# Attention in a fused attention, dense and routed expert kernel: 64-row half turns, 64-row blocks of q and k, and a new order of steps

## The reference

```python
# attention: q, k, v of shape (4, 8, 576, 64)
scores = scale * np.matmul(q, k.transpose(0, 1, 3, 2))
mask = pos[:, None] // 64 >= pos[None, :] // 64        # block causal, block 64
scores = np.where(mask, scores, -1e9)
attn = np.exp(scores - scores.max(-1, keepdims=True))
attn = attn / (attn.sum(-1, keepdims=True) + 1e-09)
x = np.matmul(attn, v)                                 # then laid out as 2304 rows of 512
# dense layer: w_in 512 x 2048, w_out 2048 x 512
h = x @ w_in
x = np.where(h > 0, h, np.exp(np.minimum(h, 0)) - 1) @ w_out
# routed layer: rows with x @ w_skip > 0 go through one of 8 experts (512 x 1024 x 512), picked by argmax
out = x; out[r] += gate[r] * (np.maximum(x[r] @ w1[e], 0) @ w2[e])
```

## Time and profile before

| | |
|---|---|
| median of 3 runs | 821.57 us (820.05 to 821.72) |
| the profiled execution | 823.07 us |
| its span, first to last instruction | 821.0 us |
| TensorE busy | 796.7 us (97%), weight loads 661.8 us (81%) |
| DVE, ACT, POOL busy | 527.3 (64%), 341.0 (42%), 244.3 us (30%) |
| mean granted clock of TensorE | 0.992 of full speed |
| attention, about | the first 200 us of the span |

### The profile page before, as it was taken

One profiled execution on the slowest core, in us unless ns is written; L12 is line 12 of the kernel. 1 busy time (PEld: TensorE's weight loads), 2 busy tenths in 40 slices (PEclk: granted clock), 3 DMA queues, 4 the chain that ended last, 5 costly groups with the idle time before them and its releaser, 6 DMA issues.

```text
span 821.0 us, 14719 instructions
## 1 busy us (share of the span) xinstructions
PE 796.7 (97%) x4610; PEld 661.8 (81%) x4611; DVE 527.3 (64%) x1291; ACT 341.0 (42%) x830; POOL 244.3 (30%) x240
## 2 busy tenths in 40 slices
PE   6999999999999999999999999999997999999995
PEld 4777777778989988988888898889875777888884
DVE  3777777775333687588488578635656799367342
ACT  4666666654342222222322322233443676256141
POOL 3666676674560121021021012100112323213111
PEclk9999999999999999999999999999997999999999
DMA  8355565645332210200200010140342699164000
GB/s 156 108 148 145 155 157 158 179 128 170 104 105 97 87 53 28 87 21 11 77 20 20 28 51 26 52 154 26 126 140 67 216 343 345 74 225 148 20 27 8
DMA packets 102912, 88.09 MB, mean 107 GB/s; under 512 B 66676, under 2 KB 78340, under 8 KB 102736
## 3 DMA queue, kind: packets, MB, share of 16 engines
q1 hardware_dynamic: 97408, 81.89, 32.6%
q0 software_dynamic: 3056, 5.00, 1.9%
q10 hardware_dynamic: 2400, 0.59, 0.4%
HBM read 72.26 MB, written 18.34 MB: 110 GB/s over the span
## 4 chain that ended last, share of the span: by engine, by line
PE 77%; SPq 10%; issue 4%; DMA 3%; DVE 3%; ACT 1%; DVEq 1%; ACTq 0%; POOL 0%; POOLq 0%
PE h_ps L1707 12%; PE out_ps L1707 11%; PE h_ps L1708 11%; PE h_ps L1709 11%; PE out_ps L1709 11%; PE out_ps L1708 11%; SPq L229 4%; SPq L231 3%; DMA recip_rows<-r_rows 2%; PE o_ps L670 2%; PE t_ps L620 2%; SPq L268 2%; SPq L265 2%; PE out_ps L1843 1%; PE s_ps L612 1%
## 5 line engine op out<-in xcount | busy, mean ns | idle before, releaser
L1534 ACT ACTIVATE ex<-h_ps 128x384 f32<-128x384 f32 x96 | 47.2, 491 | 271.8 <-PE h_ps L1709 271.8
L1707 PE MATMUL h_ps<-xt_hi,wi_hi 128*128 128x384 f32 x384 | 131.7, 343 | 0.0
L1708 PE MATMUL h_ps<-xt_lo,wi_hi 128*128 128x384 f32 x384 | 129.8, 338 | 0.0
L1709 PE MATMUL h_ps<-xt_hi,wi_lo 128*128 128x384 f32 x384 | 129.7, 338 | 0.0
L1373 DVE TENSOR_SCALAR ex<-ex 128x384 f32<-128x384 f32 x96 | 36.1, 376 | 140.1 <-ACT ex L1534 139.0
L1707 PE MATMUL out_ps<-wo_hi,gt 128*128 128x512 f32 x288 | 114.5, 398 | 0.0
L1709 PE MATMUL out_ps<-wo_hi,gt 128*128 128x512 f32 x288 | 113.9, 396 | 0.0
L1708 PE MATMUL out_ps<-wo_lo,gt 128*128 128x512 f32 x288 | 113.3, 393 | 0.0
L520 ACT ACTIVATE prob<-s_ps,negmax 128x128 f32<-128x128 f32 (+2 forms) x144 | 77.8, 548 | 61.8 <-DVE negmax L389 56.3
L1255 DVE CUSTOM_DVE_ANT_0 x2t<-x,w_raw 128x512 bf16<-128x512 f32 x108 | 82.7, 806 | 0.4
L1151 POOL TENSOR_TENSOR xt_lo<-x_raw,xt_hi 128x384 fp32r<-128x384 f32 x20 | 28.4, 1418 | 157.2 <-ACT xt_hi L1549 157.1
(11 more groups left out here) (180 smaller groups left out, 1616.3 us busy)
## 6 DMA issues: line engine op xcount, KB each, us to landing
w_raw<-in_moe_w_dram SPq DMA_DIRECT2D x56, 512.0 KB, 5.2
attn_t<-attn_sb SPq DMA_DIRECT2D x16, 288.0 KB, 2.2
x_raw<-attn_t SPq DMA_DIRECT2D x24, 192.0 KB, 2.4
out_dram<-x SPq DMA_DIRECT2D x18, 256.0 KB, 2.2
x_rows<-x SPq DMA_DIRECT2D x18, 256.0 KB, 2.5
raw_qk<-in_q_dram SPq DMA_DIRECT2D x32, 128.0 KB, 2.5
v<-in_v_dram SPq DMA_DIRECT2D x32, 128.0 KB, 2.7
wi_raw<-in_moe_w_in_dram SPq DMA_DIRECT2D x16, 256.0 KB, 2.8
```

The lines of the kernel that those rows point to most:

```text
L1534: act.activation(ex[:, f % 2], h_ps[:, f % 2, 0:NB], ACT.Exp).then_inc(ex_done, 1)
L1707: pe.matmul(dst, stat[0], mov[0], start=start, stop=False, skip_group_check=True)
L1708: pe.matmul(dst, stat[0], mov[1], start=False, stop=False, skip_group_check=True)
L1709: return pe.matmul(dst, stat[1], mov[0], start=False, stop=stop, skip_group_check=True)
```

## The change

Every turn of 128 rows by up to 128 columns becomes two transposes of 64 rows with the 64 x 64 corner of the identity, one for rows 0 to 63 and one for rows 64 to 127; their outputs go to two banks. q and k of a pair are loaded in nine blocks of 64 rows, q on partitions 0 to 63 and k on partitions 64 to 127, so one turn of a block turns q and k together, and one transfer per head and tensor brings all 576 rows. `values` is one group of 28 products. Tile 1 and the blocks of q and k are turned into the banks of `o_ps`, everything else into `t_ps`. Tiles 0 and 3 are copied out by ACT instead of DVE; the reciprocal rows and the tail of q by DVE instead of ACT. `ready` lets TensorE's sequencer pass only when all signals of a turn are there. The steps of all engines are in a new order. The core of the diff:

```diff
-    raw = [sb(f"raw_qk{i}", [P, 2, FULL, 2, D], F32) for i in range(2)]
-    raw_tail = [sb(f"raw_tail{i}", [P, 2, D], F32) for i in range(2)]
+    raw = [sb(f"raw_qk{i}", [P, BLOCKS, 2, D], F32) for i in range(2)]
...
+    def load_blocks(eng, t, n, i, rows):
         for h in range(2):
-            eng.dma_start(dst[:, 0:FULL, h, :], heads[h, 0:FULL * P, :]
-                          .rearrange("(t p) d -> p t d", p=P)).then_inc(landed, 16)
-        eng.dma_start(tail, heads[:, FULL * P:S, :].rearrange("h s d -> s h d")).then_inc(landed, 16)
+            eng.dma_start(raw[i][rows, :, h, :], heads_of(t, n)[h].rearrange("(b p) d -> p b d", p=D))\
+               .then_inc(qk_in[i], 16)
...
     (sync: load_recips)
+            wait(sp, out_done, n)
             wait(sp, r_stored, 16 * n + 16)
...
     (sync: step)
+            if now and not (first and now[0] == 0):
+                load_wi(now[0])
+            if ahead:
+                load_qk(*ahead)
+            if now and not first:
+                load_v(*now)
+            if past:
                 store_recips(*past)
-            if (older := pair(kk, i, -2)):
+            if older:
                 store(*older)
             if past:
                 load_recips(*past)
-            if (ahead := pair(kk, i, 3)):
-                load_qk(*ahead)
-            if (after := pair(kk, i, 1)):
-                load_wi(after[0])
...
     (vector: step)
             if now:
                 row_max(now[0], 0)
                 row_max(now[0], 1)
             if past:
-                for h in range(2):
-                    turned_head(*past, 3, h)
+                recips(past[0])
+            if after:
+                tail_q(*after)
             if past:
-                recips(past[0])
+                turned_last(*past)
+            if now:
+                row_max(now[0], 2)
+            if past:
+                recip_rows(past[0])
             if older:
                 final(*older)
             if now:
                 row_max(now[0], 3)
-                turned_pair(*now, 0)
-                turned_pair(*now, 1)
+                turned_halves(*now, 1, o_turns, t1_done, t1_out)
                 row_max(now[0], LAST)
+                turned_halves(*now, 2, t_ps, t2_done, t2_out)
...
     (scalar: step)
+            if after:
+                high_q(*after)
+                high_k(*after)
+            if past:
+                guard(*past)
+                turned_first(*past)
+            if after:
+                tail_k(*after)
             if now:
                 exp(*now, 0)
                 exp(*now, 1)
+                exp(*now, 2)
+            if past:
+                turned_third(*past)
+            if now:
                 exp(*now, 3)
                 exp(*now, LAST)
...
     (tensor)
+        def ready(*waits):
+            for signal, value in waits:
+                wait(pe, signal, value)
+            hold(pe, held_pe)
+
+        def turn_rows(dst, at, src):
+            for s, rows in enumerate(HALVES):
+                last = pe.transpose(dst[0:src.shape[1], s, at:at + D], src[rows, :], ident[rows, rows])
+            return last
+
+        def turn_qk(n, i):
+            ready((qk_in[i], 64 * (n // 2) + 64), (t1_out, n - 1))
+            for b in range(2 * FULL):
+                last = turn_rows(o_turns, b * D, raw[i][:, b].rearrange("p h d -> p (h d)"))
+            last.then_inc(qk_turned, 1)
...
+        def step(kk, i, before_mixed=lambda: None):
+            scores(*now, 0)
+            scores(*now, 1)
+            turn_mixed(past, after)       # tile 0, last tile and corner of past; tail block of after
+            scores(*now, 2)
+            if older:
+                values(*older, (prep_out, 3 * now[0] + 5) if after else (t1_out, now[0]))
+            if past:
+                turn_recips(past[0])
+            scores(*now, 3)
+            if past:
+                turn_tile(past[0], 3, t_ps, t3_done, (r_row_done, past[0] + 1))
+            turn_tile(now[0], 1, o_turns, t1_done, (exp_done, exps(now[0], 1, 1)), (out_done, now[0] - 1))
+            scores(*now, LAST)
+            turn_tile(now[0], 2, t_ps, t2_done, (exp_done, exps(now[0], 2, 1)), *copied)
+            if ahead:
+                turn_qk(*ahead)
```

More of the change, by code:

```diff
@@ L74, in attention_engines @@
     PAIRS = B * H // 2
-    NK = PAIRS // 2
     GROUP = H // 2
@@ L93, in attention_engines @@
     COLS = 2 * FULL + 1
-    TURNS = 7
+    SCORES = 4
+    BLOCKS = S // D
+    HALVES = [slice(s * D, (s + 1) * D) for s in range(2)]
     WO, XT1, GT = LATER_AT
@@ L296, in sync @@
         load_wi(0)
[L297 to L300, removed]
+        for m in range(-1, 4):
+            step(m // 2, m % 2)
+        with sp.Fori(2, PAIRS // 2 - 2) as kk:
             for i in range(2):
@@ L306, in sync @@
             load_x_rows(sp, attn_t, c, 0, x_raw, x_in)
[L307 to L311, removed]
+        for m in range(PAIRS - 4, PAIRS):
+            step(m // 2, m % 2)
+        sp.wait_ge(s_done, SCORES * (PAIRS - 1))
         first_wo()
@@ L577, in scores, with turn_recips, turn_tile @@
+        def turn_recips(n):
+            ready((rec_done, n + 1), (corner_out, n + 1))
+            turn_rows(t_ps, 0, recip[:, :]).then_inc(r_turned, 1)
+        def turn_tile(n, u, dst, turned, *waits):
+            ready(*waits)
+            for h in range(2):
+                for j in range(u + 1):
+                    last = turn_rows(dst, (h * (u + 1) + j) * D, prob[u][h][:, j * P:(j + 1) * P])
+            last.then_inc(turned, 1)
         def scores(n, i, u):
@@ L602, in scores @@
             dst = s_pair(u)
-            rows = [slice(h * D, (h + 1) * D) for h in range(2)]
             mine = slice(Q + u * P, Q + (u + 1) * P)
@@ L655, in turn_corner @@
[L655 to L668 removed]
+            if u:
+                last.then_inc(s_done, 1)
@@ L669, in values @@
+        def values(n, i, *waits):
+            for signal, value in waits:
+                wait(pe, signal, value)
+            wait(pe, v_in[i], 48 * (n // 2) + 48)
+            wait(pe, out_done, n)
+            for j, a, b in PIECES:
                 for h in range(2):
-                    last = pe.matmul(o_ps[h * D:(h + 1) * D, O0 + a:O0 + b], vb[i][:, j, h, :],
+                    last = pe.matmul(o_ps[HALVES[h], O0 + a:O0 + b], vb[i][:, j, h, :],
                                      pt[i][:, h, j, a:b], start=(j == 0), stop=(j == LAST),
@@ new lines, in tensor @@
+        pe.wait_ge(const_done, 9)
+        turn_qk(0, 0)
+        turn_mixed(None, (0, 0))
+        step(0, 0, lambda: turn_qk(1, 1))
+        for m in range(1, 4):
+            step(m // 2, m % 2)
+        with pe.Fori(2, PAIRS // 2 - 1) as kk:
+            for i in range(2):
+                step(kk, i)
+        for m in range(PAIRS - 2, PAIRS):
+            step(m // 2, m % 2)
+        last, older = (PAIRS - 1, 1), (PAIRS - 2, 0)
+        turn_tile(PAIRS - 1, 3, t_ps, t3_done, (exp_done, exps(PAIRS - 1, 3, 1)), (t2_out, PAIRS))
@@ L721, in tensor @@
         pe.wait_ge(wi_lo_done, PAIRS)
-        pe.wait_ge(exp_done, exps(last[0], 3, 1))
         hidden(0)
-        for h in range(2):
-            turn_head(last[0], 3, h)
-        values(*older, 1)
-        turn_last(last[0], turned, turns(last[0], 3, 1))
-        turn_corner(last[0])
-        pe.wait_ge(rec_done, PAIRS)
-        turn_recips(last_rows)
+        pe.wait_ge(t3_out, PAIRS)
+        turn_mixed(last, None)
+        values(*older, (t1_out, PAIRS))
+        turn_recips(PAIRS - 1)
         hidden(1)
-        values(*last, 0)
```

346 lines of the change are left out of this document (127 added, 219 removed).

## The result

| | before | after |
|---|---|---|
| median of the runs, us | 821.64 (820.05 to 821.89, 4 runs) | 811.95 (810.8 to 813.89, 4 runs) |
| ratio | | 0.9888, 95% interval 0.9866 to 0.9911 |
| profiled execution, us (span) | 823.07 (821.0) | 812.12 (810.3) |
| mean granted clock | 0.992 | 0.983 |
| mean of 15 periods between reciprocals, us | 11.22 | 10.30 |

The kernel is faster by 1.1%. The sign and the range (792 to 814) held, the size did not: 22 us were forecast, 9.7 came.

A forecast was written before the change was run, and what follows sets the result against it. TensorE, busy all the time, was taken as the bound at 11.2 us a step; it would need 9.0, SyncE's queue 9.65, taken as 9.7. 15 x (11.22 - 9.7) = 22.8 us less gave 799.5 us, range 792 to 814.

The forecast's parts named there:

- The turns: TensorE in attention: two halves run side by side in 0.055 us instead of 0.109, saving 1.9 us a step.
- Rival A: TensorE's turns: halves cost as much as a whole, 0.109 us, by weight loads; 10.5 a step, 811 us; chance 0.16.
- C: TensorE's issue: four instructions a turn make it slower, 13.8 us a step, 860; chance 0.10, shared with other slower causes.
- The engines' chain: TensorE's attention step: 8.7 us of work plus 0.3 for sequencer waits, 9.0; no other engine passes 9.0.
- changes of kind: TensorE switching between 128-row and 64-row work or to products with v: 4 of 10 left, 0.6 us less a step.
- The queue becomes the bound: SyncE's queue in attention: its 9.65 us a step exceeds TensorE's 9.0, so it sets the pace.
- Rival B: SyncE's queue doesn't bind: 9.0 to 9.1 us a step, 789 us; chance 0.07.
- Rival D: A ring of waits round several engines (turn, copy, next turn): about 10.3 us a step, 808 us; chance 0.15.
- The queue's step: SyncE's queue: third q and k loads gone, 1.6 us less, 0.05 for an added wait: 9.65 us a step.
- The x rows: SyncE's queue, unrolled steps: four x row loads against a queue a few tenths faster; 9.7 us kept as mean.
- Start and end: Before the first turn and after the last pair of attention: nothing won or lost.
- The sum: Whole attention stage: 15 x (11.22 - 9.7) = 22.8 us won, passing to the end one to one.

The follow-up runs named there:

- e4: Changed kernel with every turn as one transpose of 128 rows instead of two halves: mean period 10.69 us but for one of 15.4; its total, 794.28 us, can't be compared.
- e9: e8 with the k load of each pair's second head, from pair 4 on, issued by ACT instead of SyncE: 796.16 us, ratio 0.9649.
- e1: Changed kernel with two of the four read-backs of the reciprocals left out of SyncE's queue: 799.0 us, ratio 0.9685.
- e3: Changed kernel with the v loads issued between the store of the reciprocals and their read-back: 807.15 us, ratio 0.9771.
- e8: Changed kernel with v loads between store and read-back, later x loads, and reciprocals stored in two transfers and read back in two: 797.74 us, ratio 0.9687.
- e2: Kernel before the change with two of the four read-backs of the reciprocals left out: 820.57 us, ratio 0.9941.
- e6: Changed kernel loading only four of nine blocks of q and k, still on 64 partitions: 803.1 us, timed once, total no verdict.
- e7: Changed kernel loading q and k as four blocks on all 128 partitions, the ninth block's worth left out: 790.78 us, timed once, total no verdict.
- e5: Changed kernel with the four x row loads for the next stage issued one step and a half later: 807.65 us, ratio 0.9805.

## Why the prediction was right in sign and wrong in size

*The turns.* Right. A pair of halves costs 0.066 us in the run of seven and, by the starts of the single halves in the run of eight, 0.059, forecast 0.055, price of a whole 0.109; e4 puts eight whole turns at 1.15 us. Rival A is out, and C too. The load of a half, 146 ns, stands near the 140 of a whole turn and far below the 203 of an ordinary load of as many columns. The rule of the Trainium skill (TensorE: Matmul & The Clock Gate, LDWEIGHTS) that I weighed against it, by which a half costs the load of a whole, doesn't hold for these transposes; the measurement decides. My estimate from its figure, 0.107 us a turn, is one load of 128 columns; a turn of halves has two, so by the rule it would take that only if the two run side by side. Measured are 0.059 to 0.066 for both.

*The engines' chain.* Right in its sum, in part by luck: 8.7 and 0.3 for waits gave 9.0, and steps not held by the queue are 9.0 to 9.1 (the changed kernel's second and third, e9's at 9.1). The terms were off against each other. Halves and the changes of kind that they do away with were to bring 1.9 + 0.6 = 2.5, and by e4 they bring 1.7; the new order, of which the forecast had only 0.3 lost to waits, brings 0.5. Both sums are 2.2.

*The queue becomes the bound.* Right, and shown by e1, e3 and e8 against e2: the same cut is worth 11 us in attention after the change and 0.4 before it. Rival B is out, since a queue without its excess (e9) gives 9.20. Rival D, a ring of waits among the engines at 10.3, had the right number by another cause: with the engines' order untouched, a shorter queue takes the period to 9.5 and 9.2.

*The queue's step: the term that failed.* I wrote "The third took 100.45 to 101.23 and 102.42 to 103.25: 0.78 + 0.83 = 1.6 us of issue gone", and so 9.65. I let the remaining four loads keep the price of loads onto 128 partitions. They now go onto 64, and e6 and e7 show that this alone raises two of them from 0.97 to 1.51 us. In e7, where they keep 128 partitions, the queue's step is 9.76 and the mean period 9.69, next to the 9.65 and 9.7 of the forecast. The earlier trace rows had it in view: the third load, small and onto 64 partitions, took 0.68 us, while each of the large ones took half of 0.99. Net gain 0.88 instead of 1.6, which makes 11.2 - 0.9 + 0.05 = 10.4, and the wait for the landing hardly grew (2.4 against 2.1 us in seven steps). The measured step is 10.54 in the two steps from 104.56 and 10.62 in the six from 61.93. That is 0.9 to 1.0 over the forecast, 0.7 of it by the loads onto 64 partitions; the last 0.2 is not accounted for. A reading beside it was off too, without effect: the last read-back is issued 0.9 us before the q load at 110.59, not 0.6, so it had 1.1 us to spare, not 0.8. The Trainium skill (DMA: Bandwidth & Descriptors, Rules for kernel authors) advises against two transfers to disjoint partition halves, because they share the same DMA engines, and for one onto 128 partitions. This trace agrees with the advice, by another row than that reason: the issue time on SyncE. Whether the two halves' transfers hold each other up on the DMA engines, no run here shows.

*The x rows.* Underpriced. I wrote that four loads of x rows are issued in the unrolled steps and took 9.7 as the mean. Before the change they made one period 11.62 instead of 11.2; on a queue that is already late they made it 14.5, and e5 without them there has 10.0. The halved clock after the pause is part of that price: 6.56 us instead of 4.6 from tile 1 to the next reciprocal, so 1.9 of the 14.5. The forecast knew neither that nor the half clock behind three shorter pauses.

*Start and end.* "Nothing" was wrong. The first reciprocal is 2.3 us earlier and the last 16.1, but the expert stage only 10.25: the new order puts more of the last pair's work behind its reciprocal. The first product of the next stage starts 0.3 us after that reciprocal (176.31), where it started 4.0 before it (188.04), and 56 instead of 40 products with v stand behind it, so that from it to the stage's first output product it is 13.7 us, before 12.2.

*The sum.* Forecast 22.8. Periods: 15 x (11.22 - 10.30) = 13.8, so 9.0 missing. Against 9.7 a step, the nine in the middle lose 9.4, mostly to the queue's step, and the one with the x rows 4.8; the other five, 7.9 to 9.1 each and not held by the queue, win 5.2 that I had not counted. Start and end: 16.1 - 13.8 = 2.3 won and 16.1 - 10.25 = 5.85 lost, 3.5 missing. 22.8 - 9.0 - 3.5 = 10.3 at the expert stage, 10.95 in the whole profiled execution. The half clock is in these numbers and not beside them: it follows the pauses (mean clock 0.983 after the change, 0.991 in e8 and e9), and its share of the 9.0 is not separated.

Left open: one long step (12.3 us after the change, 13.3 in e8, 10.2 in e9) where SyncE's loop begins. The queue's step there is 11.05, 11.58 and 11.42 us from wi load to wi load, since single issues take longer in it (two k loads 1.79 us instead of 1.29, in e8 the store of the result 1.49 instead of 0.38); why they do, no run shows. Open is also why a load onto 64 partitions takes longer to issue.

## What to carry to other kernels

When an engine is made faster and a queue stands at the same height, price every transfer of that queue by the shape it will have, its partitions included, from a row of a transfer of that shape; counting transfers is not enough. A wait that hides a landing is free to fill: move independent loads between the store and its read-back before taking anything away. Loads for the next stage go where the queue has room, not where their data is first ready.

## What the runs showed of the hardware

- The issue of one load of q or k by SyncE's queue took 0.60 to 0.69 us onto 64 partitions (60 to 135 us, the changed kernel and e6), with 4 or 9 blocks of 64 elements a partition alike, and 0.37 to 0.55 onto 128 (the kernel before and e7, but for one of 1.62). It is no rule for all shapes: the store of the reciprocals from 9 partitions took 0.40 to 0.51, a read-back onto 64 took 0.51 to 0.61.
- Two 64-row transposes of 64 columns run side by side, 0.059 to 0.066 us for the two at a granted clock of 1.00, and their weight loads of 128 columns (146 ns for the probabilities, 163 for q and k) don't cost what ordinary ones of 128 columns do (203 ns).
- In the changed kernel, pauses of TensorE of 3.01, 1.98, 1.64 and 1.48 us were followed by half clock (granted 0.50 from 153 to 158, 66 to 68 and 141 to 144 us, 0.59 from 86 to 88), pauses of 1.69 (twice), 1.18, 1.17 and 0.61 us by none (1.00). The length of the single pause does not tell which.
- A k load issued by ACT took 0.62 us of its queue, as on SyncE.
